# Gate logits of six token groups: row products with sums on VectorE in place of transposes and strip products on TensorE, in a fused retention, gated feed-forward and mixture-of-experts kernel

## The chip, the cores and the metric

One core of one Trainium2 chip. The metric is the device time of one execution in microseconds (us). Three timed executions of the kernel before gave 1068.44, 1069.57 and 1070.39 us; the median is 1069.57.

## The reference, cut to what matters

Three parts follow each other, in float32: a retention (linear attention with a decaying state, 4 x 8 heads x 768 steps x 64) that gives 3072 tokens of 512 numbers; a gated feed-forward layer; and eight experts, of which each token uses one.

```python
x = attention(q, k, v)                      # (3072, 512)
y = ((x @ w_a) * (x @ w_b)) @ w_out         # (3072, 512), 1536 wide inside
logits = y @ w_gate                         # (3072, 8)
e_idx = np.argmax(logits, axis=1)
gate_w = softmax(logits)[arange, e_idx]
eom = 1 / (1 + np.exp(-(y @ w_output_gate)))   # (3072, 8)
out[t] = gate_w[t] * eom[t, e_idx[t]] * (relu(y[t] @ w1[e_idx[t]]) @ w2[e_idx[t]])
```

So each token needs 16 numbers of its `y`: 8 gate logits and 8 output gate logits. They are what the change computes in another way.

## The kernel before, in words

The kernel is written instruction by instruction for each engine, with semaphores between them; each engine's order is the order of the code, and no scheduler moves anything. Three stages follow each other: attention (to about 87 us of the span), feed-forward (to about 713 us), experts.

**Feed-forward.** The tokens go in 8 groups of 384 (`GT`), 3 tiles of 128 (`TG`). The inner 1536 columns go in 12 steps f of 128 (`KF`). TensorE does `up(g, s, f)` (L940 to L954, 24 matmuls on line L952: x times w_b, then x times w_a, each split into high and low parts), then `down(g, f - 1)` (L956 to L972, 9 matmuls on L970). `up` of step f is issued before `down` of step f - 1, so that the other engines have the length of one `up` and one `down` to make the gated product. Per step ScalarE copies b from PSUM (L712), VectorE multiplies `g_sb` = a * b (L896), ScalarE rounds it to `g_hi` (L715), VectorE subtracts `g_lo` (L898). `down` of step f waits for `g_lo` of step f, and `up` of step f for `g_sb` of step f - 2. At f = 3 the next group's x is split (`split_x_hi` L695 on ScalarE, `split_x_lo` L700 on VectorE, four instructions on L703). At a group's end ScalarE copies the three tiles of y to `y_sb` (L733), and SP stores them (L691). SP loads the next x (`load_x`, L290) at a group's start.

**Gate logits.** `y_sb` has tokens on partitions, and a matmul with the gate weights contracts over partitions, so y is transposed first. For the group before, one piece is put between `up` and `down` of each step (L977 to L985): at f = 0, 1, 2 `pe_yT` (L746, four transposes of a tile into bank 7), each copied to `yT_sb` by `dve_yT` (L771); at f = 3 `pe_partial` (L756: four matmuls, one for each 128 rows of the gate weights, each into a strip of 32 partitions), copied by `dve_partial`; at f = 4 `pe_logits` (L765, which adds the four strips and turns the result), copied by `dve_logits` to `L3`, 128 tokens x 3 tiles x 16. This happens for groups 0 to 6, each during the group after it. The last group has its own place in the expert stage.

**Routing.** Short chains of small VectorE instructions on `L3`, each waiting for the one before it (`link`, L801): `dve_choose` (f = 6, 7 instructions), `dve_gate` (f = 7, 6), `dve_scale` (f = 8, 6), `dve_rank` (f = 9, 5). ScalarE gives two exponentials, TensorE two matmuls at f = 8 (`pe_rank`).

Group 0 is apart (it also splits the weights), groups 1 to 6 run in one loop on SP, ScalarE and VectorE (two groups per turn), and group 7 is apart (it also prepares the experts). TensorE's code is unrolled.

## Time and profile before

| | |
|---|---|
| median of 3 timed runs | 1069.57 us (1068.44 to 1070.39) |
| the profiled execution, device time | 1067.78 us |
| its span, first to last instruction | 1066.0 us |
| granted TensorE clock, mean | 0.998 of full speed |
| TensorE (PE) busy | 1042.6 us, 98% |
| VectorE (DVE) busy | 407.7 us, 38% |
| ScalarE (ACT) busy | 293.4 us, 28% |
| share of TensorE in the chain that ended last | 94% |
| DMA, mean over the span | 93 GB/s |

A busy time is the union of an engine's instructions; matmuls overlap, so the mean duration of one (337 ns on L952) is longer than the time from one start to the next. The chain that ended last is followed back from the last instruction, at each step to what released it. "x24" is a run of 24 instructions merged into one row.

### The profile page before, as it was taken

What the parts mean: (1) busy time and instruction counts of PE and PEld (TensorE: products, weight loads), DVE (VectorE), ACT (ScalarE), POOL (GpSimd) and SP (SyncE); (2) the same over time, 40 slices, a digit from 0 to 9 for tenths busy, and PEclk for the clock granted to TensorE, in tenths of its full rate; (3) what the DMA queues carried; (4) which work ended last, traced back from release to release, by engine and by line L of the source; (5) the groups of instructions that cost most, each with busy time, mean ns of one, the idle gap of its engine ahead of it and who ended that gap; (6) DMA issues with size and microseconds to landing.
All of it is one profiled execution on the core that took longest, in us unless ns stands there. A gap on an engine that the chain in (4) does not pass through costs nothing.

```text
span 1066.0 us, 18259 instructions
## 1 busy us (share of the span) xinstructions
PE 1042.6 (98%) x6489; PEld 932.6 (87%) x6490; DVE 407.7 (38%) x800; ACT 293.4 (28%) x550; POOL 110.8 (10%) x108
## 2 busy tenths in 40 slices
PE   6999999999999999999999999999899999999997
PEld 5888999999999999999999999998688888888886
DVE  3445432222223223223223212458445445354542
ACT  2444332212112112122122121331334334243431
POOL 4770000000000000000000000000121111111111
PEclk9999999999999999999999999999999999999999
DMA  9997801001001001001001002200744433335311
GB/s 364 363 336 224 200 1 61 1 1 60 1 1 60 1 1 60 1 1 60 1 20 41 1 30 79 79 21 32 276 144 146 176 116 118 115 132 198 115 35 35
DMA packets 34091, 98.69 MB, mean 93 GB/s; under 512 B 4397, under 2 KB 10797, under 8 KB 34032
## 3 DMA queue, kind: packets, MB, share of 16 engines
q1 hardware_dynamic: 28976, 83.17, 23.1%
q0 software_dynamic: 4480, 13.90, 3.8%
q8 instruction: 43, 0.70, 0.3%
q10 hardware_dynamic: 576, 0.79, 0.2%
q14 instruction: 16, 0.13, 0.0%
HBM read 80.54 MB, written 18.09 MB: 93 GB/s over the span
## 4 chain that ended last, share of the span: by engine, by line
PE 94%; DMA 4%; DVE 1%; issue 1%; ACT 0%; POOL 0%; ACTq 0%; DVEq 0%; POOLq 0%
PE bank L952 38%; PE bank L970 19%; PE bank L1310 13%; PE bank L1287 13%; PE bank L1295 2%; PE bank L580 2%; DMA rows<-in_steps 2%; PE bank L633 1%; PE bank L531 1%; DMA xg<-x_dram,idx_gather 1%; PE bank L545 1%; PE bank L753 1%; PE bank L566 1%; DMA qdec_t<-in_consts 1%; PE bank L762 1%
## 5 line engine op out<-in xcount | busy, mean ns | idle before, releaser
L952 PE MATMUL bank<-x_hi,wab_hi 128*128 128x384 f32 x768 | 258.6, 337 | 0.0
L952 PE MATMUL bank<-x_hi,wab_lo 128*128 128x384 f32 x768 | 258.2, 336 | 0.0
L952 PE MATMUL bank<-x_lo,wab_hi 128*128 128x384 f32 x768 | 257.6, 335 | 0.0
L896 DVE TENSOR_TENSOR g_sb<-bank,b_sb 128x384 f32<-128x384 f32 x96 | 53.5, 557 | 368.6 <-PE bank L952 368.6
L952 PEld LDWEIGHTS bank<-x_hi,wab_hi 128*128 128x128 f32 x768 | 144.7, 188 | 3.9 <-issue 0.2
L952 PEld LDWEIGHTS bank<-x_lo,wab_hi 128*128 128x128 f32 x768 | 144.5, 188 | 3.7
L952 PEld LDWEIGHTS bank<-x_hi,wab_lo 128*128 128x128 f32 x768 | 144.4, 188 | 0.0
L1287 PE MATMUL bank<-w,xe_hi 128*128 (+1 forms) x432 | 136.2, 397 | 1.2 <-DVE xe_lo L642 1.1
L712 ACT COPY b_sb<-bank 128x384 f32<-128x384 f32 x96 | 46.3, 482 | 255.3 <-PE bank L952 255.3
L970 PE MATMUL bank<-wo_hi,g_hi 128*128 128x512 f32 x288 | 116.0, 403 | 0.0
L970 PE MATMUL bank<-wo_hi,g_lo 128*128 128x512 f32 x288 | 113.7, 395 | 0.0
L970 PE MATMUL bank<-wo_lo,g_hi 128*128 128x512 f32 x288 | 113.5, 394 | 0.0
L715 ACT CAST g_hi<-g_sb 128x384 fp32r<-128x384 f32 x96 | 49.2, 513 | 209.7 <-DVE g_sb L896 209.7
L1233 POOL DMA_INDIRECT xg<-x_dram,idx_gather x28 | 29.0, 1035 | 672.9 <-DVE idx_gather L875 630.0
L1287 PEld LDWEIGHTS bank<-w,xe_hi 128*128 128x128 f32 x432 | 78.8, 188 | 17.3 <-issue 2.1
L1310 PE MATMUL bank<-w_hi,hT_hi 128*128 (+1 forms) x216 | 86.9, 402 | 1.3 <-DVE hT_lo L1030 1.3
L1310 PE MATMUL bank<-w_hi,hT_lo 128*128 (+1 forms) x216 | 84.5, 391 | 0.0
L1287 PE MATMUL bank<-w,xe_lo 128*128 (+1 forms) x216 | 84.5, 391 | 0.0
L1310 PE MATMUL bank<-w_lo,hT_hi 128*128 (+1 forms) x216 | 84.2, 390 | 0.0
L898 DVE TENSOR_TENSOR g_lo<-g_sb,g_hi 128x384 fp32r<-128x384 f32 x96 | 53.6, 558 | 55.6 <-ACT g_hi L715 55.6
L970 PEld LDWEIGHTS bank<-wo_hi,g_hi 128*128 128x128 f32 x288 | 54.2, 188 | 13.8 <-issue 4.4
L970 PEld LDWEIGHTS bank<-wo_hi,g_lo 128*128 128x128 f32 x288 | 54.2, 188 | 11.9
(161 smaller groups left out, 1114.3 us busy)
## 6 DMA issues: line engine op xcount, KB each, us to landing
raw<-in_w SPq DMA_DIRECT2D x64, 512.0 KB, 4.8
rows<-in_steps SPq DMA_DIRECT2D x20, 768.0 KB, 7.8
rows<-in_steps SPq DMA_DIRECT2D x24, 256.0 KB, 7.3
wab_raw<-in_weights SPq DMA_DIRECT2D x24, 256.0 KB, 7.7
x_dram<-y_sb SPq DMA_DIRECT2D x8, 768.0 KB, 4.0
xT_dram<-x_all SPq DMA_DIRECT2D x6, 768.0 KB, 11.9
x_raw<-xT_dram SPq DMA_DIRECT2D x6, 768.0 KB, 5.3
wo_raw<-in_weights SPq DMA_DIRECT2D x4, 768.0 KB, 10.0
```

The source lines that it names most:

```text
L531: ins = nc.tensor.matmul(bank[2 * i + o][:, cols], kT[half_p, cols], qT[half_p, cols], start=True, stop=True)
L580: ins = nc.tensor.matmul(out_at(i, p, o), rows[:, c, 3, h * D:(h + 1) * D], probs[j][:, i, h, :], start=False, stop=(i == ROUND - 1 and p ...
L712: nc.scalar.copy(b_sb[:, f % 2], bank[2 * (f % 2) + 1][:, 0:GT]).then_inc(b_read, 1)
L715: nc.scalar.copy(g_hi[:, f % 2], g_sb[:, f % 2]).then_inc(g_hi_done, 1)
L896: nc.vector.tensor_tensor(g_sb[:, f % 2], bank[2 * (f % 2)][:, 0:GT], b_sb[:, f % 2], ALU.mult).then_inc(g_done, 1)
L898: nc.vector.tensor_tensor(g_lo[:, f % 2], g_sb[:, f % 2], g_hi[:, f % 2].bitcast(F32), ALU.subtract).then_inc(g_lo_done, 1)
L952: ins = nc.tensor.matmul(bank[to][:, 0:GT], wab(w, f, j), x[s][:, k, :], start=(k == 0 and m == 0), stop=(k == KD - 1 and m == 2))
L970: ins = nc.tensor.matmul(bank[4 + t], gp[:, f % 2, toks], wo(w, f), start=(f == 0 and m == 0), stop=(f == KF - 1 and m == 2))
L1233: nc.gpsimd.indirect_dma_start(out=xg_first[s] if i < FIRST else xg[s], out_offset=None, in_=x_dram[0:rows_there], in_offset=bass.Indirect ...
L1287: ins = nc.tensor.matmul(bank[o], x[:, s, k, :], w[:, bass.ds(half + (k * FE + o * 512), 512)], start=(k == 0 and m == 0), stop=(k == KD - ...
L1295: ins = nc.tensor.transpose(bank[2 + o][:, k * P:(k + 1) * P], h_sb[:, (4 * o + k) * P:(4 * o + k + 1) * P], ident)
L1310: ins = nc.tensor.matmul(bank[5 + s], h[:, k, :], w[:, bass.ds(half + k * DM, DM)], start=(k == 0 and m == 0), stop=(k == KE - 1 and m == 2))
```

## The change

For token groups 0 to 5, whose logits are computed during groups 1 to 6 (the loop), TensorE no longer takes part. The two outputs of each token are sums over 512 products of its row of y with a row of gate weights, and VectorE computes these directly: `dve_dots` issues 48 instructions per group (16 gate columns e x 3 tiles t), each multiplying the tile `y_sb[:, t]` (128 x 512) by `gate_row`, writing the products away and their sum to one column of `L3`. `DOTS_AT` says how many of the 48 follow each step f: none, 6, 6, 3, 6, 3, 5, 6, 6, 6, 1, none. Each waits for the one two places before it (`dots_done`); the first of each gate column waits for its row.

The gate weights must lie on all partitions for this. In group 0 TensorE transposes the gate weights once (into bank 7), VectorE copies them to `gates_T`, and SP stores them as 16 rows of 512 numbers in the part of `xT_dram` that groups 0 and 1 don't use. In each loop group SP then copies each of the 16 rows to all 128 partitions (256 KB each), through four slots `gate_row`; a row from the fifth on waits until the three products that used its slot are done. The first four stand ahead of `load_x` in SP's queue, the rest behind it.

The steps of routing move: `dve_choose` from f = 6 to 5 (it needs the first 24 products only), `seen` counts from f = 7 to 6, `dve_rank` stays at 9, the output gate (`dve_own_gate`) is at f = 10 and `dve_scale` at 11; ScalarE's two exponentials move to f = 6 and 11. `g_lo` now lies in the place of `g_sb`, so `g_sb` waits for `down` of step f - 2. ScalarE's copy of y at a group's end waits for all 48 products. Group 6 (during group 7) and group 7 keep the way of before.

```diff
--- before.py
+++ after.py
@@ -38,6 +38,9 @@
 PAIRS_MAX = (SLOT_TILES - 1) // 2
 READY = 2
 PARTS = 4
+GATE_SLOTS = 4
+DOTS = 2 * NE * TG
+DOTS_AT = (0, 6, 6, 3, 6, 3, 5, 6, 6, 6, 1, 0)
 PW = KD * FE // PARTS
 W1_SPAN, W2_SPAN = 2 * KD * FE, KE * DM
 
@@ -180,15 +183,23 @@
     small_end = at[0]
     at[0] = small_at
     b_sb = place("b_sb", (P, 2, GT))
+    g_sb_at = at[0]
     g_sb = place("g_sb", (P, 2, GT))
     g_hi = place("g_hi", (P, 2, GT), F32R)
-    g_lo = place("g_lo", (P, 2, GT), F32R)
+    g_lo = place("g_lo", (P, 2, GT), F32R, where=g_sb_at)
+    product_at = at[0]
+    at[0] += 2 * GT * 4
     y_sb = place("y_sb", (P, TG, DM))
     yT_sb_at = at[0]
     yT_sb = place("yT_sb", (P, KD, GT))
     x_raw_at = max(at[0], yT_sb_at + 3 * DM * 4)
     part_sb = place("part_sb", (P, GT), where=x_raw_at + KD * GT * 4)
     x_raw = place("x_raw", (P, TG, KD, P), where=x_raw_at)
+    after_x = x_raw_at + KD * GT * 4
+    gate_row = [place(f"gate_row{n}", (P, DM), where=(yT_sb_at, yT_sb_at + DM * 4, yT_sb_at + 2 * DM * 4, after_x)[n])
+                for n in range(GATE_SLOTS)]
+    products = [place(f"products{n}", (P, DM), where=(product_at, after_x + DM * 4)[n]) for n in range(2)]
+    gates_T = place("gates_T", (P, P), where=after_x + DM * 4)
 
     at[0] = x_raw_at
     id_first = place("id_first", (P, TILES - TG))
...
@@ -605,6 +619,7 @@
 
     AT_PART, AT_LOGITS = TG, TG + 1
     AT_CHOOSE, AT_GATE, AT_SCALE, AT_RANK = 6, 7, 8, 9
+    DOT_CHOOSE, DOT_SEEN, DOT_RANK, DOT_GATE, DOT_SCALE = 5, 6, 9, 10, 11
     LINKS = 19
     AT_FIRST = 10
     AT_W1_HI = {5: (0, 1), 6: (2, 3)}
@@ -672,13 +687,32 @@
             sp.dma_start(raw[:, q * PW:(q + 1) * PW],
                          src[bass.ds(e, 1), :, q * PW:(q + 1) * PW].rearrange("a p c -> (a p) c")).then_inc(into[q], 16)
 
+    gate_rows = x_groups[0].rearrange("p c -> (p c)")[0:2 * NE * DM].rearrange("(e k p) -> k e p", e=2 * NE, k=KD)
+    gate_rows_flat = x_groups[0].rearrange("p c -> (p c)")[0:2 * NE * DM].rearrange("(e c) -> e c", e=2 * NE)
+
+    def store_gates_T(sp):
+        sp.wait_ge(gates_T_read, 1)
+        for k in range(KD):
+            at_k = k * (P // KD)
+            sp.dma_start(gate_rows[k], gates_T[at_k:at_k + 2 * NE]).then_inc(gates_T_out, 16)
+        sp.wait_ge(gates_T_out, 16 * KD)
+
+    def load_gate_rows(sp, g, which):
+        for e in which:
+            if e >= GATE_SLOTS:
+                sp.wait_ge(dots_done, DOTS * (g - 1) + TG * (e - GATE_SLOTS + 1))
+            sp.dma_start(gate_row[e % GATE_SLOTS], gate_rows_flat[e:e + 1].to_broadcast([P, DM])).then_inc(row_in[e % GATE_SLOTS], 16)
+
     def sp_ff(sp):
         def group(g, s, first, last):
             if first:
                 sp_weights(sp)
+                store_gates_T(sp)
             elif not last:
                 sp.wait_ge(x_lo_done, KD * (g + 1))
+                load_gate_rows(sp, g, range(GATE_SLOTS))
                 load_x(sp, g + 1)
+                load_gate_rows(sp, g, range(GATE_SLOTS, 2 * NE))
             else:
 
                 for half in range(2):
@@ -720,15 +754,17 @@
                 if last and f in AT_W1_HI:
                     split_w1(act, True, 0, AT_W1_HI[f])
                 if not first:
-                    if f == AT_GATE:
+                    if f == (AT_GATE if last else DOT_SEEN):
                         act_exp(act, g - 1)
-                    if f == AT_SCALE:
+                    if f == (AT_SCALE if last else DOT_SCALE):
                         act_exp_og(act, g - 1)
             if last:
                 split_w2(act, True, 0, (0, 1, 2))
             act.wait_ge(down_done, KF * (g + 1) + 2)
             if not first:
                 act.wait_ge(x_out, 16 * g)
+                if not last:
+                    act.wait_ge(dots_done, DOTS * g)
             for t in range(TG):
                 nc.scalar.copy(y_sb[:, t, :], bank[4 + t]).then_inc(y_read, 1)
 
@@ -742,20 +778,23 @@
         act.wait_ge(og_done, g + 1)
         nc.scalar.activation(g_oge, g_og, ACT.Exp, scale=-1.0).then_inc(oge_done, 1)
 
+
+    def on_pe(g):
+        return g - (GROUPS - 2)
 
     def pe_yT(pe, g, t):
         pe.wait_ge(y_read, TG * g + t + 1)
         if t == 0:
             pe.wait_ge(rank_read, g + 1)
         else:
-            pe.wait_ge(yT_read, TG * g + t)
+            pe.wait_ge(yT_read, TG * on_pe(g) + t)
         for k in range(KD):
             ins = nc.tensor.transpose(bank[7][:, k * P:(k + 1) * P], y_sb[:, t, k * P:(k + 1) * P], ident)
         ins.then_inc(yT_done, 1)
 
     def pe_partial(pe, g, yT=yT_sb):
 
-        pe.wait_ge(yT_read, TG * (g + 1))
+        pe.wait_ge(yT_read, TG * (on_pe(g) + 1))
         pe.sem_inc(waited, 1)
         for k in range(KD):
             strip = slice(k * (P // KD), (k + 1) * (P // KD))
...
@@ -809,7 +849,10 @@
 
         v = nc.vector
         tiles = bass.ds(g * TG, TG)
-        dve.wait_ge(logit_read, TG * (g + 1) + 1)
+        if isinstance(g, int) and on_pe(g) >= 0:
+            dve.wait_ge(logit_read, TG * (on_pe(g) + 1))
+        else:
+            dve.wait_ge(dots_done, DOTS * g + DOTS // 2)
         link(v.tensor_reduce(g_max, L3[:, :, 0:NE], AX.X, ALU.max))
         v.tensor_tensor(g_sub, L3[:, :, 0:NE], over(g_max, NE), ALU.subtract).then_inc(sub_done, 1)
         link(v.tensor_tensor(g_eq, L3[:, :, 0:NE], over(g_max, NE), ALU.is_equal))
@@ -819,10 +862,18 @@
         link(v.tensor_copy(onehot[:, tiles, :], g_key8))
 
     def dve_gate(dve, g, link):
-
+        dve_own_gate(dve, g, link)
+        dve_seen(dve, g, link)
+
+    def dve_own_gate(dve, g, link):
         v = nc.vector
+        if not (isinstance(g, int) and on_pe(g) >= 0):
+            dve.wait_ge(dots_done, DOTS * (g + 1))
         link(v.tensor_tensor(g_og8, g_key8, L3[:, :, NE:2 * NE], ALU.mult))
         v.tensor_reduce(g_og, g_og8, AX.X, ALU.add).then_inc(og_done, 1)
+
+    def dve_seen(dve, g, link):
+        v = nc.vector
         link(v.tensor_copy(seen[:, 0, :], seen[:, TG, :]))
         for t in range(TG - 1):
             link(v.tensor_tensor(seen[:, t + 1, :], seen[:, t, :], g_key8[:, t, :], ALU.add))
@@ -883,6 +934,20 @@
         ins.then_inc(first_slots_done, 1)
 
     ROUTE_STEPS = {AT_CHOOSE: dve_choose, AT_GATE: dve_gate, AT_SCALE: dve_scale, AT_RANK: dve_rank}
+    DOT_STEPS = {DOT_CHOOSE: dve_choose, DOT_SEEN: dve_seen, DOT_RANK: dve_rank, DOT_GATE: dve_own_gate, DOT_SCALE: dve_scale}
+
+    def dve_dots(dve, g, f):
+
+        for n in range(sum(DOTS_AT[:f]), sum(DOTS_AT[:f + 1])):
+            e, t = n // TG, n % TG
+            if e == 0:
+                dve.wait_ge(y_read, TG * g + t + 1)
+            if t == 0:
+                dve.wait_ge(row_in[e % GATE_SLOTS], 16 * (2 * NE // GATE_SLOTS * g + e // GATE_SLOTS + 1))
+            if n > 1:
+                dve.wait_ge(dots_done, DOTS * g + n - 1)
+            nc.vector.scalar_tensor_tensor(products[n % 2], y_sb[:, t], 1.0, gate_row[e % GATE_SLOTS], ALU.mult, ALU.mult,
+                                           accum_out=L3[:, t, e:e + 1]).then_inc(dots_done, 1)
 
     def dve_ff(dve):
         first_link = linker(dve, 0, first_linked)[0]
@@ -893,6 +958,7 @@
                 n = g * KF + f
                 dve.wait_ge(a_done, n + 1)
                 dve.wait_ge(b_read, n + 1)
+                dve.wait_ge(down_done, n - 1 + 2)
                 nc.vector.tensor_tensor(g_sb[:, f % 2], bank[2 * (f % 2)][:, 0:GT], b_sb[:, f % 2], ALU.mult).then_inc(g_done, 1)
                 dve.wait_ge(g_hi_done, n + 1)
                 nc.vector.tensor_tensor(g_lo[:, f % 2], g_sb[:, f % 2], g_hi[:, f % 2].bitcast(F32),
@@ -901,7 +967,16 @@
                     split_x_lo(dve, g + 1, 1 - s)
                 if first and f + 2 < KF:
                     split_w_lo(dve, f + 2)
-                if not first:
+                if first and f == 0:
+                    dve.wait_ge(gates_T_done, 1)
+                    nc.vector.tensor_copy(gates_T, bank[7][:, 0:P]).then_inc(gates_T_read, 1)
+                if not first and not last:
+                    dve_dots(dve, g - 1, f)
+                    if f in DOT_STEPS:
+                        DOT_STEPS[f](dve, g - 1, link[0])
+                        if f == DOT_SCALE:
+                            assert link[1][0] == LINKS, link[1]
+                if last:
                     if f < TG:
                         dve_yT(dve, g - 1, f)
                     elif f == AT_PART:
...
@@ -974,15 +1048,17 @@
         def group(g, s, first, last):
             for f in range(KF):
                 up(g, s, f)
-                if not first:
+                if first and f == 0:
+                    nc.tensor.transpose(bank[7][:, 0:P], gates_pad.rearrange("p k e -> p (k e)"), ident).then_inc(gates_T_done, 1)
+                if last:
                     if f < TG:
                         pe_yT(pe, g - 1, f)
                     elif f == AT_PART:
                         pe_partial(pe, g - 1)
                     elif f == AT_LOGITS:
                         pe_logits(pe, g - 1)
-                    elif f == AT_SCALE:
-                        pe_rank(pe, g - 1)
+                if not first and f == AT_SCALE:
+                    pe_rank(pe, g - 1)
                 if last and f == AT_FIRST:
                     pe_first_slots(pe)
                 if last and f == KF - 1:
...
```

Left out of the diff are the new semaphores and a constant that is taken off the counts of those semaphores that now count fewer groups (`on_pe`).

TensorE, the end of `up` at f = 0 and the start of `up` at f = 1 in group 1 (L952 is `up`, L753 `pe_yT`). Before:

```order
L952 MATMUL bank<-x_lo,wab_hi 128x384
L952 MATMUL bank<-x_hi,wab_lo 128x384
L753 MATMUL bank<-ident,y_sb 128x128 [waits rank_read,y_read]
L753 MATMUL bank<-ident,y_sb 128x128 x3
L952 MATMUL bank<-x_hi,wab_hi 128x384 [waits g_done]
L952 MATMUL bank<-x_lo,wab_hi 128x384
```

After the change, at the same place (`up` is on L1026):

```order
L1026 MATMUL bank<-x_lo,wab_hi 128x384
L1026 MATMUL bank<-x_hi,wab_lo 128x384
L1026 MATMUL bank<-x_hi,wab_hi 128x384 [waits g_done]
L1026 MATMUL bank<-x_lo,wab_hi 128x384
```

The four transposes are gone, and so are those at f = 1 and 2, the strips at f = 3 and the three matmuls at f = 4.

VectorE, step f = 9 of a loop group, where `dve_rank` follows. Before:

```order
L896 TENSOR_TENSOR g_sb<-bank,b_sb 128x384 [waits b_read,a_done]
L898 TENSOR_TENSOR g_lo<-g_sb,g_hi 128x384 [waits g_hi_done]
L848 TENSOR_TENSOR g_5_65<-bank,g_3_63 128x24 [waits rank_done]
L851 TENSOR_REDUCE g_5_71<-g_5_65 128x3 [waits rank_read]
```

After the change (L962 and L964 make `g_sb` and `g_lo`, L949 is one product with sum, L899 begins `dve_rank`):

```order
L962 TENSOR_TENSOR g_sb<-bank,b_sb 128x384 [waits down_done,b_read,a_done]
L964 TENSOR_TENSOR g_lo<-g_sb,g_hi 128x384 [waits g_hi_done]
L948 REGISTER_ALU
L949 SCALAR_TENSOR_TENSOR products_116,L_59<-y_sb,gate_row_112 128x512 [waits dots_done]
L948 REGISTER_ALU [waits row_in2]
L949 SCALAR_TENSOR_TENSOR products_115,L_59<-y_sb,gate_row_113 128x512 [waits dots_done]
...
L948 REGISTER_ALU [waits row_in3]
L949 SCALAR_TENSOR_TENSOR products_116,L_59<-y_sb,gate_row_114 128x512 [waits dots_done]
L948 REGISTER_ALU
L949 SCALAR_TENSOR_TENSOR products_115,L_59<-y_sb,gate_row_114 128x512 [waits dots_done]
L899 TENSOR_TENSOR g_5_65<-bank,g_3_63 128x24 [waits rank_done]
L902 TENSOR_REDUCE g_5_71<-g_5_65 128x3 [waits rank_read]
```

Six products stand ahead of `dve_rank`, and `g_sb` of the next step comes behind both.

SP, the start of group 1. Before:

```order
L291 ISA [waits x_lo_done]
L291 DMA x_raw<-xT_dram 128x1536
L690 REGISTER_ALU
L691 ISA [waits y_read]
L691 DMA x_dram<-y_sb 128x3x512
```

After the change:

```order
L704 DMA gate_row_111<-xT_dram 128x512 [waits x_lo_done]
L704 DMA gate_row_112<-xT_dram 128x512
L704 DMA gate_row_113<-xT_dram 128x512
L704 DMA gate_row_114<-xT_dram 128x512
L302 ISA
L302 DMA x_raw<-xT_dram 128x1536
L703 ISA
L704 DMA gate_row_111<-xT_dram 128x512 [waits dots_done]
L703 REGISTER_ALU
L704 DMA gate_row_112<-xT_dram 128x512 [waits dots_done]
```

Four rows stand ahead of `x_raw`, and twelve more, each waiting for products, ahead of the store of y.

## Rows read from the trace of the kernel before

**Rows 1.** Page: each engine's busy time, share of span and instructions.

```profile
PE 1042.6 (98%) x6489; PEld 932.6 (87%) x6490; DVE 407.7 (38%) x800; ACT 293.4 (28%) x550; POOL 110.8 (10%) x108
```

**Rows 2.** Page: the chain that ended last, shares by line.

```profile
PE bank L952 38%; PE bank L970 19%; PE bank L1310 13%; PE bank L1287 13%; PE bank L1295 2%; PE bank L580 2%; DMA rows<-in_steps 2%; PE bank L633 1%; PE bank L531 1%; DMA xg<-x_dram,idx_gather 1%; PE bank L545 1%; PE bank L753 1%; PE bank L566 1%; DMA qdec_t<-in_consts 1%; PE bank L762 1%
```

**Rows 3.** Busy in a middle group: length, PE, PEld, DVE, ACT, POOL, clock, DMA.

```profile
315.93:394.43 78.50, 78.50 (x427) 72.88 (x427) 21.24 (x57) 15.39 (x33) 0.00 (x0) 1.00 0.06 21
```

**Rows 4.** The chain in order of time (start, us, what).

```profile
315.93 4.14 PE bank L970 x18
320.06 4.19 PE bank L952 x24
...
394.43 4.16 PE bank L970 x18
```

**Rows 5.** Timeline of VectorE over one middle group (start, us, what).

```profile
324.29 0.56 DVE L896 TENSOR_TENSOR g_sb<-bank,b_sb 128x384 f32<-128x384 f32 x1 [6.63 <-PE bank L952]
325.42 0.56 DVE L898 TENSOR_TENSOR g_lo<-g_sb,g_hi 128x384 fp32r<-128x384 f32 x1 [0.58 <-ACT g_hi L715]
325.90 0.68 DVE L773 COPY yT_sb<-bank 128x512 f32<-128x512 f32 x1
328.90 0.56 DVE L896 TENSOR_TENSOR g_sb<-bank,b_sb 128x384 f32<-128x384 f32 x1 [2.32 <-PE bank L952]
...
335.60 0.56 DVE L896 TENSOR_TENSOR g_sb<-bank,b_sb 128x384 f32<-128x384 f32 x1 [4.40 <-PE bank L952]
...
342.30 0.56 DVE L896 TENSOR_TENSOR g_sb<-bank,b_sb 128x384 f32<-128x384 f32 x1 [4.41 <-PE bank L952]
...
343.91 1.96 DVE L703 TENSOR_TENSOR x_lo<-x_raw,x_hi 128x384 fp32r<-128x384 f32 x4
...
349.54 0.56 DVE L896 TENSOR_TENSOR g_sb<-bank,b_sb 128x384 f32<-128x384 f32 x1 [3.20 <-PE bank L952]
...
356.46 0.56 DVE L896 TENSOR_TENSOR g_sb<-bank,b_sb 128x384 f32<-128x384 f32 x1 [5.11 <-PE bank L952]
...
362.72 0.56 DVE L896 TENSOR_TENSOR g_sb<-bank,b_sb 128x384 f32<-128x384 f32 x1 [4.57 <-PE bank L952]
...
364.34 0.17 DVE L813 TENSOR_REDUCE g<-L 128x3 f32<-128x24 f32 x1
...
365.62 0.18 DVE L819 COPY onehot<-g 128x24 f32 x1
...
375.26 0.56 DVE L896 TENSOR_TENSOR g_sb<-bank,b_sb 128x384 f32<-128x384 f32 x1 [3.58 <-PE bank L952]
...
381.94 0.56 DVE L896 TENSOR_TENSOR g_sb<-bank,b_sb 128x384 f32<-128x384 f32 x1 [3.77 <-PE bank L952]
```

**Rows 6.** Busy by line and shape, VectorE.

```profile
L898 DVE TENSOR_TENSOR g_lo<-g_sb,g_hi 128x384 fp32r<-128x384 f32 x96 | 53.6, 558 | 55.6 <-ACT g_hi L715 55.6
...
L329 DVE TENSOR_TENSOR wo_lo<-wo_raw,wo_hi 128x512 fp32r<-128x512 f32 x12 | 8.2, 684 | 3.7 <-ACT wo_hi L315 3.7
```

**Rows 7.** Timeline of VectorE in the attention stage.

```profile
29.64 2.48 DVE L490 TENSOR_TENSOR probs<-bank,mask_t 128x512 f32<-128x512 f32 x4 [3.60 <-PE bank L531]
```

**Rows 8.** Timeline of ScalarE: y to SBUF at a group's end.

```profile
320.10 1.56 ACT L733 COPY y_sb<-bank 128x512 f32<-128x512 f32 x3 [3.03 <-PE bank L970]
```

**Rows 9.** DMA issues: KB each, median us to landing.

```profile
rows<-in_steps SPq DMA_DIRECT2D x24, 256.0 KB, 7.3
...
x_dram<-y_sb SPq DMA_DIRECT2D x8, 768.0 KB, 4.0
...
x_raw<-xT_dram SPq DMA_DIRECT2D x6, 768.0 KB, 5.3
```

More of the change, by code:

```diff
@@ L599, in build @@
     waited = sem("waited")
+    gates_T_done, gates_T_read, gates_T_out, dots_done = (sem("gates_T_done"), sem("gates_T_read"), sem("gates_T_out"),
+                                                          sem("dots_done"))
+    row_in = [sem(f"row_in{n}") for n in range(GATE_SLOTS)]
     x_out = sem("x_out")
@@ L765, in pe_logits @@
     def pe_logits(pe, g, part=part_sb):
-        pe.wait_ge(part_read, g + 1)
+        pe.wait_ge(part_read, on_pe(g) + 1)
         for t in range(TG):
@@ L771, in dve_yT @@
     def dve_yT(dve, g, t):
-        dve.wait_ge(yT_done, TG * g + t + 1)
+        dve.wait_ge(yT_done, TG * on_pe(g) + t + 1)
         nc.vector.tensor_copy(yT_sb[:, :, t * P:(t + 1) * P], bank[7].rearrange("p (k t) -> p k t", k=KD)).then_inc(yT_read, 1)
     def dve_partial(dve, g, part=part_sb):
-        dve.wait_ge(part_done, g + 1)
+        dve.wait_ge(part_done, on_pe(g) + 1)
         nc.vector.tensor_copy(part, bank[7][:, 0:GT]).then_inc(part_read, 1)
     def dve_logits(dve, g):
-        dve.wait_ge(logit_done, TG * (g + 1))
+        dve.wait_ge(logit_done, TG * (on_pe(g) + 1))
         nc.vector.tensor_copy(L3.rearrange("p t e -> p (t e)"), bank[7][:, 0:TG * 2 * NE]).then_inc(logit_read, TG)
@@ L785, in pe_rank @@
         pe.wait_ge(seen_done, g + 1)
-        pe.wait_ge(logit_read, TG * (g + 1) + 1)
+        if on_pe(GROUPS - 2) <= (on_pe(g) if isinstance(g, int) else -1):
+            pe.wait_ge(logit_read, TG * (on_pe(g) + 1))
         to = bank[7][:, 0:TG * NE]
@@ L934, in pe_ff @@
         pe.sem_inc(down_done, 2)
-        pe.sem_inc(logit_read, 1)
         pe.sem_inc(rank_read, 1)
@@ L1015, in pe_counts @@
         pe.wait_ge(seen_done, GROUPS)
-        pe.wait_ge(logit_read, TG * GROUPS + 1)
+        pe.wait_ge(logit_read, TG * (on_pe(LAST) + 1))
         nc.tensor.matmul(bank[7][:, COUNT:COUNT + NE], ones_t, seen[:, TG, :], start=True, stop=True)
@@ L1040, in dve_route @@
         for t in range(TG):
-            dve.wait_ge(yT_done, TG * LAST + t + 1)
+            dve.wait_ge(yT_done, TG * on_pe(LAST) + t + 1)
             v.tensor_copy(yT_last[:, :, t * P:(t + 1) * P], bank[4 + t].rearrange("p (k t) -> p k t", k=KD)).then_inc(yT_read, 1)
```

## Prediction

> **What bounds the kernel now.** I read the page first: TensorE is busy 98% of the span [rows 1], and the chain that ended last runs through `up` (L952, 38%) and `down` (L970, 19%), with L753 (`pe_yT`) and L762 (`pe_partial`) in it at 1% each [rows 2]. Those two are what the change takes away in six groups. Then one middle group: the 78.50 us from 315.93 to 394.43 are all TensorE busy at clock 1.00, while VectorE is busy for 21.24 and DMA 6% [rows 3]. The chain in order of time repeats with the same period: `down` at 315.93 and again at 394.43 [rows 4]. In such a group time is gained only by taking instructions off TensorE, and VectorE has 57 us to spare, if nothing waits for it.
>
> **What is removed.** The cost of each inserted piece is read from VectorE's `g_sb`, which starts when `up` of its step ends [rows 5]. A step without insert takes 362.72 - 356.46 = 6.26 us: 4.19 for `up` [rows 4], the rest, 2.07, for `down`. From f = 0 to f = 1 there is only one `up` and the first tile's transposes: 328.90 - 324.29 = 4.61, so 0.42 for them. The other two tiles: 335.60 - 328.90 and 342.30 - 335.60, each 6.70, so 0.44 each. The strips: 349.54 - 342.30 = 7.24, so 0.98. The logits: 356.46 - 349.54 = 6.92, so 0.66. Sum 2.94 us. The rank matmuls (381.94 - 375.26 = 6.68, so 0.42) stay. Twelve plain steps, 75.1, with 2.94 and 0.42 make 78.5, the measured period. Six groups give 6 x 2.94 = 17.6 us. The period would be 75.56.
>
> **What is added on TensorE.** One transpose in group 0: a quarter of 0.44, and the stop and restart of the stream. I take 0.2 us. VectorE's copy of it (128 columns) and SP's four stores lie in group 0, where SP has only y to store afterwards; nobody waits for them before the first row is loaded. Zero.
>
> **What is added on VectorE, and when it shows.** The cover is large: `down` of step f needs `g_lo` of step f one plain step, 6.26 us, after the end of `up` f. `g_lo` is ready 1.69 us after `g_sb` starts (325.42 + 0.56 - 324.29), and the next instruction can start at 1.61 (325.90) [rows 5]. So VectorE may be some 4.5 us late before TensorE stands. With a time d from the start of one product to that of the next, a step of six products takes 1.61 + 6d.
>
> No row shows the new instruction. The nearest is the two-source subtraction of 128 x 512 float32, both sources in SBUF like here: 684 ns, against 558 for 384 columns, so 0.98 ns per column [rows 6]. Back to back they overlap: four 512-column products take 2.48 us, so (2.48 - 0.68) / 3 = 0.60 us from start to start [rows 7]. What the sum costs more is unknown. If it comes for nothing, d = 0.60; that is the low end, since every column must still pass. If it is like one more small instruction behind each product, the routing chain prices it: seven from 364.34 to 365.62 + 0.18, 1.46 us, 0.21 each [rows 5]; d = 0.81. If nothing overlaps, 0.684 + 0.17 = 0.85. The high end is a product at half rate: 512 more column times, 0.60 + 0.50 = 1.10, and 1.20 if the whole time doubles. I take 0.75, between the first two, because columns, types and places are those of the 684 ns row.
>
> The longest path through VectorE: f = 1 to 10 without a gap are 10 x 1.61 = 16.1, the 48 products, the four `x_lo` (1.96, from 343.91, less overlap: 1.9), and the routing steps that stay there: `dve_choose` 1.46 and eleven small ones (`seen` 4, rank 5, output gate 2) at 0.21, 3.8. Then f = 11 to the next f = 1 hang on TensorE: `g_sb` and `g_lo` 1.69, `down` 2.07, two `up` 8.38, together 12.1. Sum: 33.9 + 48d. It sets the period only beyond 75.56, that is from d = 0.87; it eats the whole gain (78.5) from d = 0.93. At 0.75 it is 69.9. The densest steps, f = 7, 8 and 9, take 1.61 + 4.5 = 6.1 each at d = 0.75, and 1.0 more at f = 9 for the rank: some 0.9 us late against a cover of 4.5. Hence zero. What is queued behind a product is `g_sb` of the next step; ScalarE's `g_hi` and TensorE's `down` wait for that. The exponentials, moved to f = 6 and 11, find their inputs made a step earlier or, at 11, lie behind `g_hi`. `g_lo` in the place of `g_sb` adds a wait for `down` f - 2, which TensorE issues before the `up` for which `g_sb` waits anyway. The three copies of y that go, 0.68 us each [rows 5], are in steps that the products fill again. If the cover were gone, a dense step would cost what it takes over 6.26 us.
>
> **DMA and SP.** Sixteen rows of 256 KB are 4.2 MB per group, 55 GB/s on queues that are 6% busy now [rows 3]. At the start y is in SBUF at 320.10 + 1.56 = 321.7 [rows 8]; then SP issues the store of y (768 KB, 4.0 us), rows 0 to 3 and x (5.3 us when alone) [rows 9]. The first product wants its row at f = 1, about 330.1, 8.4 us later; if 768 KB need 5.3 us, the store and the first two rows need 8.8 in line, inside 8.4 and the cover. x comes some 7 us later than before, at about 334 to 338; it is wanted at 342. Later rows are asked for nine products ahead; in the dense steps two rows are used per 6.26 us through four slots, so a slot turns in 12.5 us, of which 2.3 are its products. A row may need 10 us. A 256 KB load in the crowded first stage took 7.3 [rows 9]. Zero.
>
> **Sum.** Against the profiled execution, 1067.78: -17.6 + 0.2 gives 1050.4. The median of the timed runs lies 1.8 above the profiled one, 1069.57, so I expect 1052.2.
>
> **The rivals.**
>
> *Products at half rate.* The mechanism: two float32 streams from SBUF and a running sum, one column in two cycles. For it speaks only that no row shows this instruction; against it, that two float32 sources without a sum run at 0.98 ns per column [rows 6]. Then d = 1.10 to 1.20, VectorE is the engine that TensorE waits for in steps 6 to 12, and the period is 33.9 + 48d = 86.7 to 91.5: 6 x 8.2 = 49 to 6 x 13.0 = 78 us more, 1119 to 1148. It decides from d = 0.93 on. The Trainium skill states this very rule: in "Vector Engine (DVE) Microarchitecture Reference", points that are easy to get wrong, this instruction form "with two non-bf16 SBUF sources halves throughput". By that rule the result would be 1119 or more. Nothing in this trace shows whether it holds, and the form without a sum does not show the halving. Chance 0.17, and 0.02 for other ways to over 1072.
>
> *The sum as a second instruction, dearer than taken, or rows late.* With d between 0.87 and 0.93 the gain shrinks by 48 x 0.01 x 6 = 2.9 us for each 0.01. Rows that need 13 us, like a crowded queue, would miss by 3 us at each of two turns of a slot in the dense steps, less the 4.5 of cover: 1.5 us a group, 9 in all, 1061. For it: 96 copies with one source address each, a pattern that the trace lacks. Against it: idle queues. Range 1055 to 1067, chance 0.07. That the sum is a second instruction is what the Trainium skill says ("VectorE: DVE Perf Modes", two Vector instructions with no wait between them: "an op that also writes out its accumulator is two instructions"); by that d would be 0.81 here, and the result still 1052.
>
> *The gain is not one.* The removed pieces could stand where TensorE would have waited for `g_lo`. The rows speak against it: `g_lo` is ready 4.5 us early [rows 5], and TensorE shows no idle time [rows 3]. Then 1067 to 1072, chance 0.04.
>
> **How the numbers follow.** Hidden products: chance 0.70, 1052.2 with 1050 to 1055. Partly hidden: 0.07. No gain: 0.04. Slower: 0.19. A measurement of this kernel tells 0.2%, some 2 us, from no change. The range leaves out the half rate and reaches over the others: 1049.5 to 1068. Faster 0.77, same 0.04, slower 0.19.
>
> **What would show each step right or wrong.** Right: the chain repeats every 75.5 to 75.6 us; from f = 0 to 1 `g_sb` takes 4.2 and all other steps but f = 9 6.26; L753's count falls from 84 to 12. L949 has 288 instructions of 0.65 to 0.85 us. VectorE's busy time in a group is 21.2 - 2.0 + 48 x 0.75, about 55. `down` never waits for `g_lo`. Rows land within 10 us. Wrong: products over 1 us, or an idle time of TensorE before L1044 released by `g_lo`, late in the group (half rate); the first product of a step waiting for a row, with the same idle time behind it (late rows); the period at 75.6 but a longer time elsewhere, in group 0 or the experts, which I price at nothing.

## The result, and the profile after

The changed kernel took 1053.11 us (median of 4 runs, 1050.76 to 1054.60), the kernel before 1069.98 in the same comparison (4 runs, 1068.44 to 1072.87). The ratio is 0.9837, 95% interval 0.9807 to 0.9868: 1.6% faster. Forecast were 1052.2 in a range of 1049.5 to 1068.0. The profiled execution took 1050.76 us against 1050.4 forecast for it, with a span of 1048.9, 17.1 less than before.

The engines, from the page (before: [rows 1]):

```profile
PE 1026.0 (98%) x6334; PEld 920.8 (88%) x6335; DVE 571.3 (54%) x1347; ACT 293.4 (28%) x550; POOL 110.7 (11%) x108
```

TensorE lost 16.6 us of busy time, VectorE gained 163.6, and the end followed TensorE.

One middle group of the changed kernel, to be read like [rows 3] (length; busy time of PE, PEld, DVE, ACT, POOL; clock; DMA share; GB/s):

```profile
310.34:385.92 75.58, 75.58 (x401) 70.86 (x401) 48.47 (x148) 15.40 (x33) 0.00 (x0) 1.00 0.24 77
```

Its length fell from 78.50 to 75.58 us, still filled by TensorE, with VectorE at 48.47 in place of 21.24 and DMA at 24% in place of 6%. The chain in order of time shows the period as in [rows 4]: `down` (now L1044) of f = 10 and 11 at 310.34, 385.92, 461.48 and 537.06, and behind the first of these two `up` without anything between them:

```profile
310.34 4.16 PE bank L1044 x18
314.49 8.34 PE bank L1026 x48
...
385.92 4.14 PE bank L1044 x18
...
461.48 4.16 PE bank L1044 x18
...
537.06 4.18 PE bank L1044 x18
```

VectorE's rows for the new instruction (busy by line and shape: busy us, mean ns, idle time before):

```profile
L949 DVE SCALAR_TENSOR_TENSOR products<-y_sb,gate_row 128x512 f32<-128x512 f32 x288 | 180.9, 688 | 0.0
...
L949 DVE DVE_READ_ACCUMULATOR products<-y_sb,gate_row 128x1 f32 x288 | 24.2, 84 | 0.0
```

The product with sum is two instructions: the product, 688 ns where the plain subtraction of the same shape has 684 [rows 6], and the reading of the sum, 84 ns. Where they fall is seen in VectorE's timeline of one group, from f = 0 to 1 and from f = 8 to 10, where the products are densest (`g_sb` of f = 0, 1, 8, 9, then two products of f = 9, the first and last of the rank steps, and `g_sb` of f = 10):

```profile
318.71 0.56 DVE L962 TENSOR_TENSOR g_sb<-bank,b_sb 128x384 f32<-128x384 f32 x1 [5.45 <-PE bank L1026]
...
322.88 0.56 DVE L962 TENSOR_TENSOR g_sb<-bank,b_sb 128x384 f32<-128x384 f32 x1 [2.46 <-PE bank L1026]
...
366.74 0.56 DVE L962 TENSOR_TENSOR g_sb<-bank,b_sb 128x384 f32<-128x384 f32 x1 [0.89 <-PE bank L1026]
...
373.42 0.56 DVE L962 TENSOR_TENSOR g_sb<-bank,b_sb 128x384 f32<-128x384 f32 x1 [1.31 <-PE bank L1026]
...
375.03 0.69 DVE L949 SCALAR_TENSOR_TENSOR products<-y_sb,gate_row 128x512 f32<-128x512 f32 x1
375.64 0.08 DVE L949 DVE_READ_ACCUMULATOR products<-y_sb,gate_row 128x1 f32 x1
375.64 0.69 DVE L949 SCALAR_TENSOR_TENSOR products<-y_sb,gate_row 128x512 f32<-128x512 f32 x1
...
378.71 0.18 DVE L899 TENSOR_TENSOR g<-bank,g 128x24 f32<-128x24 f32 x1
...
379.56 0.17 DVE L905 TENSOR_SCALAR t_tle<-g_ranki 128x3 int32 x1
379.95 0.56 DVE L962 TENSOR_TENSOR g_sb<-bank,b_sb 128x384 f32<-128x384 f32 x1 [0.22 <-DVE t_tle L905]
```

`g_sb` of f = 1 starts 4.17 us behind that of f = 0 (4.61 in [rows 5]), with no transposes between. At f = 9 the next product starts together with the reading of the sum before it, 0.61 us behind the last one. Behind six products and the rank steps, which end at 379.56 + 0.17, `g_sb` of f = 10 starts at 379.95; a plain step after 373.42 is 379.69, so it is 0.26 late. That is all the lateness in the group, against a cover of 4.5.

The transfers (KB each, median us to landing):

```profile
gate_row<-xT_dram SPq DMA_DIRECT2D x96, 256.0 KB, 3.2
...
x_raw<-xT_dram SPq DMA_DIRECT2D x6, 768.0 KB, 6.8
```

A row of gate weights lands in 3.2 us (6.1 at most); x, which has four of them ahead, in 6.8 in place of 5.3 [rows 9].

### The profile page after: what moved, and what is told of

Its sections match the earlier page's. It is cut to its first block, busy times and chain, and to the rows that moved or that the text cites. A ratio compares the mean times of both kernels' runs of the same rounds, so it can differ in the third digit from the quotient of the medians.

```text
span 1048.9 us, 18935 instructions
## 1 busy us (share of the span) xinstructions
PE 1026.0 (98%) x6334; PEld 920.8 (88%) x6335; DVE 571.3 (54%) x1347; ACT 293.4 (28%) x550; POOL 110.7 (11%) x108
## 4 chain that ended last, share of the span: by engine, by line
PE 94%; DMA 4%; DVE 1%; issue 1%; POOL 0%; ACT 0%; ACTq 0%; DVEq 0%; POOLq 0%
PE bank L1026 38%; PE bank L1044 19%; PE bank L1386 14%; PE bank L1363 13%; PE bank L1371 2%; PE bank L591 2%; DMA rows<-in_steps 2%; PE bank L542 1%; PE bank L648 1%; DMA xg<-x_dram,idx_gather 1%; PE bank L556 1%; DMA qdec_t<-in_consts 1%; PE bank L577 1%; PE bank L932 0%; POOL out L1314 0%
## 5 line engine op out<-in xcount | busy, mean ns | idle before, releaser
L1026 PE MATMUL bank<-x_hi,wab_hi 128*128 128x384 f32 x768 | 257.8, 336 | 0.0
L1026 PE MATMUL bank<-x_hi,wab_lo 128*128 128x384 f32 x768 | 257.7, 336 | 0.0
L1026 PE MATMUL bank<-x_lo,wab_hi 128*128 128x384 f32 x768 | 257.2, 335 | 0.0
L949 DVE SCALAR_TENSOR_TENSOR products<-y_sb,gate_row 128x512 f32<-128x512 f32 x288 | 180.9, 688 | 0.0
L962 DVE TENSOR_TENSOR g_sb<-bank,b_sb 128x384 f32<-128x384 f32 x96 | 53.5, 558 | 186.3 <-PE bank L1026 185.0
L1026 PEld LDWEIGHTS bank<-x_hi,wab_hi 128*128 128x128 f32 x768 | 144.3, 188 | 4.3 <-issue 0.4
L1026 PEld LDWEIGHTS bank<-x_lo,wab_hi 128*128 128x128 f32 x768 | 144.2, 188 | 3.7
L1026 PEld LDWEIGHTS bank<-x_hi,wab_lo 128*128 128x128 f32 x768 | 144.1, 188 | 0.0
L1044 PE MATMUL bank<-wo_hi,g_lo 128*128 128x512 f32 x288 | 114.3, 397 | 0.0
L1044 PE MATMUL bank<-wo_lo,g_hi 128*128 128x512 f32 x288 | 114.2, 396 | 0.0
L1044 PE MATMUL bank<-wo_hi,g_hi 128*128 128x512 f32 x288 | 113.9, 396 | 0.0
L964 DVE TENSOR_TENSOR g_lo<-g_sb,g_hi 128x384 fp32r<-128x384 f32 x96 | 53.6, 558 | 55.7 <-ACT g_hi L749 55.7
L1044 PEld LDWEIGHTS bank<-wo_hi,g_lo 128*128 128x128 f32 x288 | 54.4, 189 | 11.8
```

Source lines behind the costliest of these rows:

```text
L949: nc.vector.scalar_tensor_tensor(products[n % 2], y_sb[:, t], 1.0, gate_row[e % GATE_SLOTS], ALU.mult, ALU.mult, accum_out=L3[:, t, e:e + ...
L962: nc.vector.tensor_tensor(g_sb[:, f % 2], bank[2 * (f % 2)][:, 0:GT], b_sb[:, f % 2], ALU.mult).then_inc(g_done, 1)
L964: nc.vector.tensor_tensor(g_lo[:, f % 2], g_sb[:, f % 2], g_hi[:, f % 2].bitcast(F32), ALU.subtract).then_inc(g_lo_done, 1)
L1026: ins = nc.tensor.matmul(bank[to][:, 0:GT], wab(w, f, j), x[s][:, k, :], start=(k == 0 and m == 0), stop=(k == KD - 1 and m == 2))
L1044: ins = nc.tensor.matmul(bank[4 + t], gp[:, f % 2, toks], wo(w, f), start=(f == 0 and m == 0), stop=(f == KF - 1 and m == 2))
```

## The experiments

Ten runs follow, each beside the kernel before; e9 is the changed kernel once more, and e10 that of e2. The two theories at the start: (T) the gain is TensorE's own time in the removed pieces, and the products are free because VectorE may be 4.5 us late and is not; (R) some of the gain, or a hidden price, is elsewhere: in the copies and waits that went, in VectorE's total, or in the rows. A period is the mean over the six loop groups, taken from ScalarE's first copies of y at the groups' ends.

### e1: TensorE's pieces put back

```diff
+    def pe_idle_pieces(pe, g, f):
+        if f < TG:
+            pe.wait_ge(y_read, TG * g + f + 1)
...
+            for k in range(KD):
+                nc.tensor.transpose(bank[7][:, k * P:(k + 1) * P], y_sb[:, f, k * P:(k + 1) * P], ident)
+        elif f == AT_PART:
+            for k in range(KD):
+                nc.tensor.matmul(bank[7][k * (P // KD):(k + 1) * (P // KD), 0:GT], gates_pad[:, k, :], y_sb[:, k % TG, 0:GT], start=True, stop=True)
+        elif f == AT_LOGITS:
+            for t in range(TG):
+                nc.tensor.matmul(bank[7][:, t * 2 * NE:(t + 1) * 2 * NE], y_sb[:, t, 0:P], sel, start=True, stop=True)
```

> The changed kernel with TensorE's pieces put back where they stood, as work that nobody reads: in the six loop groups 12 transposes of y at f = 0 to 2, four strip products of 384 columns at f = 3 and three of 16 columns at f = 4; VectorE still makes all logits as row products. Theory (the whole gain is TensorE's own time, the products cost nothing): the group period goes back from 75.57 to 78.5 us, 6 x 2.94 = 17.6 us more than the changed kernel, so the time of the kernel before, ratio 0.999 to 1.001. Rival (part of the gain is the waits and copies that went with the pieces, or the products cost something hidden): period clearly off 78.5; 77 or less if the copies carried part of the gain, 79 or more if the products cost something as soon as TensorE has its old work.

Measured: 1068.98 us (12 runs), before 1067.44, ratio 1.0007 (0.9992 to 1.0022). The period is 78.53, against 78.52 in the kernel before; two `down` of the chain:

```profile
316.47 4.14 PE bank L1059 x18
...
394.97 4.16 PE bank L1059 x18
```

So the gain is the time of those matmuls, as far as this comparison can tell. The copies of VectorE that went with them carried no part of it (they are not put back here), and 288 products, 96 row loads and one more transpose together cost less than it can tell: 0.02 us in the period, and at most 0.22% of the whole time by the interval.

### e4 and e5: how late may VectorE be?

```diff
-DOTS_AT = (0, 6, 6, 3, 6, 3, 5, 6, 6, 6, 1, 0)
+DOTS_AT = (0, 6, 6, 3, 6, 3, 5, 14, 4, 0, 1, 0)
```

> The changed kernel with 14 products at f = 7, 4 at f = 8, none at f = 9 in place of 6, 6, 6. The step f = 7 then takes VectorE 1.61 + 14 x 0.613 = 10.2 us against 6.26, so g_sb of f = 8 starts some 4 us late. Theory (cover of 4.5 us until down waits): no change of the time, period 75.57. Rival (a VectorE that is over its step costs TensorE what it is over): 3.9 us per group, 23 us in all.

Measured: 1051.52 us, ratio 0.9835 (0.9809 to 0.9861), period 75.60, the same as the changed kernel's. `g_sb` of f = 7 and of f = 8:

```profile
363.66 0.56 DVE L962 TENSOR_TENSOR g_sb<-bank,b_sb 128x384 f32<-128x384 f32 x1 [0.82 <-PE bank L1026]
...
373.84 0.55 DVE L962 TENSOR_TENSOR g_sb<-bank,b_sb 128x384 f32<-128x384 f32 x1
```

They are 10.18 us apart where a plain step has 6.26: 3.9 us late in every group, and nothing lost. The rival would have cost 23.

In e5 the line reads `5, 18, 0, 0, 1, 0` from f = 6 on.

> The changed kernel with 18 products at f = 7 and none at f = 8 and 9 in place of 6, 6, 6. Step f = 7 takes VectorE 1.61 + 18 x 0.613 = 12.6 us, so g_sb of f = 8 starts 6.4 us late and g_lo with it. Theory (cover of 4.5 us): TensorE waits once per group for g_lo of f = 8, some 1.6 to 1.9 us, 9 to 11 us in all, 1062 to 1064. Rival (no cover): 6.4 us per group, 38 us in all. Rival (more cover than the rows show): no change.

Measured: 1063.02 us, ratio 0.9954 (0.9938 to 0.9971), period 77.32. VectorE, `g_sb` of f = 7 and 8 and `g_lo` of f = 8, then the first `down` of f = 8 on TensorE:

```profile
363.54 0.56 DVE L962 TENSOR_TENSOR g_sb<-bank,b_sb 128x384 f32<-128x384 f32 x1 [0.82 <-PE bank L1026]
...
376.18 0.55 DVE L962 TENSOR_TENSOR g_sb<-bank,b_sb 128x384 f32<-128x384 f32 x1
...
377.31 0.56 DVE L964 TENSOR_TENSOR g_lo<-g_sb,g_hi 128x384 fp32r<-128x384 f32 x1 [0.58 <-ACT g_hi L749]
```

```profile
377.92 0.50 PE L1044 MATMUL bank<-wo_hi,g_hi 128*128 128x512 f32 x1 [1.47 <-DVE g_lo L964]
```

12.64 us apart, 6.4 late, and TensorE stands 1.47 us until `g_lo`; with the stream's restart the period grows by 1.73 (77.33 against 75.60). Of 6.4 us late, some 4.6 were covered, which is the cover read from [rows 5].

### e6 and e7: how many products fit?

```diff
-            if n > 1:
-                dve.wait_ge(dots_done, DOTS * g + n - 1)
-            nc.vector.scalar_tensor_tensor(products[n % 2], y_sb[:, t], 1.0, gate_row[e % GATE_SLOTS], ALU.mult, ALU.mult,
-                                           accum_out=L3[:, t, e:e + 1]).then_inc(dots_done, 1)
+            for r in range(TIMES[e % 2]):
+                c = dots_before(e) + t * TIMES[e % 2] + r
+                if c > 1:
+                    dve.wait_ge(dots_done, DOTS * g + c - 1)
+                nc.vector.scalar_tensor_tensor(products[c % 2], y_sb[:, t], 1.0, gate_row[e % GATE_SLOTS], ALU.mult, ALU.mult,
+                                               accum_out=L3[:, t, e:e + 1] if r == 0 else again[:, c % 2:c % 2 + 1]).then_inc(dots_done, 1)
```

`TIMES` is (1, 2) in e6 and (2, 2) in e7.

> The changed kernel with every product of an odd gate column made twice, the second sum to a place that nobody reads: 72 products per group in place of 48. Theory (the path through VectorE from f = 1 to 10 and back over TensorE, 33.9 + 0.613 x 72 = 78.0 us, sets the period as soon as it is over 75.57): period 78 to 79, some 15 to 21 us more than the changed kernel, 1068 to 1074. Rival (only VectorE's sum per group counts): busy 48.5 + 24 x 0.61 = 63.1 us of 75.6, no change.

Measured: 1071.89 us, ratio 1.0045 (1.0028 to 1.0062), period 78.97. A middle group:

```profile
320.05:398.94 78.89, 76.06 (x402) 70.77 (x401) 62.63 (x196) 14.97 (x34) 0.00 (x0) 1.00 0.24 74
```

VectorE is busy for 62.63 of 78.89 us and sets the period all the same: TensorE stands for 2.8 us of the group.

> The changed kernel with every product made twice, 96 per group, which is also what products at half the rate would have cost. Theory (path 33.9 + 0.613 x 96 = 92.7 us): period 92 to 94, 103 to 109 us more than the changed kernel, 1156 to 1162. Rival (only VectorE's sum counts): busy 77.9 us and 7 of waits for g_hi, period at most 85, at most 57 us more.

Measured: 1164.5 us (2 runs), ratio 1.0909 (1.0887 to 1.0931), period 94.3. A middle group:

```profile
257.14:352.29 95.15, 82.28 (x402) 73.75 (x401) 77.33 (x244) 14.53 (x34) 0.00 (x0) 0.95 0.19 62
```

This is the half rate that was the rival on the slow side, made by hand. The path through VectorE gives 78.0 and 92.7, and the periods are 78.97 and 94.3; VectorE's total gives no change and at most 85, and is refuted. The path is somewhat short. Of e7's times, 1164.5 us lies above the 1156 to 1162 that were expected. The group shown has the granted clock at 0.95, and the rows say where: at its end TensorE stands for 3.66 us, and the 18 `down` behind that take 7.26 us in place of 4.16:

```profile
344.91 7.26 PE bank L1053 x18
...
344.90:349.00 4.10, 4.09 (x10) 0.50 0.00 0
```

The second line is a stretch on TensorE alone (its length, busy, granted clock, DMA share, GB/s). The formula has no term for that. What makes up the 1.0 us of e6, whose clock stays at 1.00, was not tried.

### e3 and e8: fewer slots for the rows

```diff
-GATE_SLOTS = 4
+GATE_SLOTS = 2
```

> The changed kernel with two slots for gate rows in place of four. Theory: a slot turns in three products (1.84 us) and a load of 3.2 us with its issue, some 5.4 us in all, below the 6.26 us in which a dense step uses each slot once, so VectorE waits for no row at a step's start and little within it, and the time stays that of the changed kernel within 1 us. Rival (four slots are what hides the rows): rows come late in the dense steps by more than the cover of 4.5 us, and the period grows by 1 us or more, 6 us or more in all.

Measured: 1051.93 us, ratio 0.9839 (0.9813 to 0.9864), period 75.60. VectorE does wait for rows, 4.1 us in one group (who waited for whom: us in total, times, longest). One such wait is at f = 7, whose `g_sb` starts at 364.39; that of f = 8 starts at 371.22, 0.57 later than a plain step. With two more such waits and the rank steps `g_sb` of f = 10 starts at 385.85, some 2.3 us late:

```profile
DVE products L949 <- DMA gate_row<-xT_dram: 4.1, 3, 1.5
```

```profile
369.99 0.69 DVE L949 SCALAR_TENSOR_TENSOR products<-y_sb,gate_row 128x512 f32<-128x512 f32 x1 [1.45 <-DMA gate_row<-xT_dram]
...
371.22 0.55 DVE L962 TENSOR_TENSOR g_sb<-bank,b_sb 128x384 f32<-128x384 f32 x1
...
385.85 0.56 DVE L962 TENSOR_TENSOR g_sb<-bank,b_sb 128x384 f32<-128x384 f32 x1 [0.22 <-PE bank L1044]
```

The cover takes it all: the period is that of the changed kernel. With four slots VectorE waits for no row.

> The changed kernel with one slot for gate rows: each row is asked for when the three products of the row before are done, so every load of some 3.6 us stands on VectorE's path. Theory: 16 x 1.84 + 15 x 3.6 = 83.4 us for the rows, with f = 11 to f = 1 behind it (12.1) and the first step's 1.6, a period of about 97, some 130 us more than the changed kernel, 1180 or so. Rival (the loads overlap with the rest of VectorE's and TensorE's steps): period below 85.

Measured: 1224.41 us (2 runs), ratio 1.147 (1.1411 to 1.1529), period 104.1 where 97 were expected. Two rows in the chain, and one row's products on VectorE (its first, the `g_sb` between its second and third, and the first of the next row):

```profile
278.84 2.98 DMA gate_row<-xT_dram
...
283.89 3.11 DMA gate_row<-xT_dram
```

```profile
335.92 0.69 DVE L949 SCALAR_TENSOR_TENSOR products<-y_sb,gate_row 128x512 f32<-128x512 f32 x1 [3.24 <-DMA gate_row<-xT_dram]
...
337.14 0.55 DVE L962 TENSOR_TENSOR g_sb<-bank,b_sb 128x384 f32<-128x384 f32 x1
...
342.58 0.69 DVE L949 SCALAR_TENSOR_TENSOR products<-y_sb,gate_row 128x512 f32<-128x512 f32 x1 [3.14 <-DMA gate_row<-xT_dram]
```

The load itself is as short as before, 3 us. A pause for a row is 3.1 to 3.3 in these rows, not 3.6: in this group (103.1 us) the twelve plain turns from row to row take 5.04 to 5.33 us where the sum had 5.44, which makes it 3.5 us shorter. What the sum left out is more than that, and is of two kinds.

The first is seen in the second fence: where a row's products lie on both sides of a step's end, the 1.61 us of `g_sb` and `g_lo` stand ahead of the third one, and the next load is asked for later. Four step ends in a group are such (f = 6 to 9), 6.4 us; the routing steps at two of them, `seen` and rank, add some 2.

The second is on TensorE. Before the last 18 `down` of the group it stands for 5.33 us, and then runs at granted clock 0.50, so that they take 6.07 us in place of 4.16:

```profile
363.99 6.07 PE bank L1044 x18
...
363.90:367.00 3.10, 3.02 (x7) 0.50 0.00 0
```

Hence the way from `g_sb` of f = 11 over TensorE to that of the next f = 1 takes 13.4 us in place of 12.1. Together this makes up the 6 us between 97.1 and this group's 103.1 within some tenths. It is a reading of the trace; no run tests a part of it by itself.

### e2, e9 and e10: the seventh group as well

If VectorE may be late, group 7 has room for products as well: e2 makes those of group 6 there. TensorE's and VectorE's old pieces there are gone, ScalarE's second exponential is at f = 10, and `dve_scale` follows the first slots.

```diff
+DOTS_LAST = (0, 7, 7, 7, 7, 7, 3, 4, 4, 2, 0, 0)
...
+                load_gate_rows(sp, g, range(GATE_SLOTS))
                 for half in range(2):
                     sp.wait_ge(a_done, g * KF + 2 * half + 2)
                     load_expert(sp, raw1, w1_in, 0, raw1_in, (2 * half, 2 * half + 1))
+                    load_gate_rows(sp, g, range(4 + 4 * half, 8 + 4 * half))
...
-        return g - (GROUPS - 2)
+        return g - (GROUPS - 1)
...
+                    dve_dots(dve, g - 1, f, DOTS_LAST)
+                    for step in {6: (dve_choose,), 7: (dve_seen,), 9: (dve_rank, dve_own_gate)}.get(f, ()):
+                        step(dve, g - 1, link[0])
```

> The changed kernel with group 6 treated like groups 0 to 5: its 48 products are made during group 7, at 7 per step for f = 1 to 5 and 3, 4, 4, 2 for f = 6 to 9; no y transposes, strips or logit matmuls in group 7; the output gate at f = 9, the scale at f = 10. Theory (cover of 4.5 us against a product every 0.61 us): another 2.94 us less, about 1050.2 by the median of 1053.1, ratio to before 0.981. Rival (group 7's VectorE, which also splits the first expert's weights and finds its first slots, has no room): TensorE waits for g_lo or for the first slots at f = 10, and the gain is nil or a loss of some us.

Measured: 1045.33 us (before 1067.44), ratio 0.9803 (0.9778 to 0.9828). Group 7 fell from 82.99 to 78.46 us, that is by 4.53 and not 2.94. It has VectorE at 58.26 us:

```profile
615.65:694.11 78.46, 78.46 (x429) 73.77 (x428) 58.26 (x163) 20.37 (x37) 2.21 (x2) 1.00 0.39 125
```

The other 1.6 us are the clock behind the 21 narrow matmuls for the first slots (L881 before, 2 columns each), which end at 704.7 us in the kernel before, at 687.4 in the changed kernel and at 683.2 in e2. TensorE in the kernel before (stretch, its length, busy, granted clock, DMA share, GB/s):

```profile
702.00:704.50 2.50, 2.50 (x25) 1.00 0.00 0
704.50:707.50 3.00, 3.00 (x12) 0.75 0.00 0
707.50:710.00 2.50, 2.50 (x11) 0.62 0.42 116
```

In the changed kernel:

```profile
685.00:687.40 2.40, 2.40 (x23) 1.00 0.00 0
687.40:691.20 3.80, 3.80 (x12) 0.55 0.01 4
691.20:695.40 4.20, 4.20 (x26) 1.00 0.46 125
```

In e2, at the same place:

```profile
680.70:683.20 2.50, 2.50 (x24) 1.00 0.00 0
683.20:685.40 2.20, 2.20 (x11) 1.00 0.00 0
```

In the first two the clock falls to its lower level, 1.2 GHz, for some 3 us (0.55 over 3.8 us), and the nine matmuls of `down` at 687.40 take 3.75 us in place of 2.08; in e2 they take 2.17. To see whether that is chance, the changed kernel and that of e2 were run again side by side.

> The changed kernel unaltered, timed beside e10 on one chip, with a new profile. Theory: ratio to before 0.984, group period 75.57. Open is group 7: in the first profile down of f = 9, which follows the 21 narrow matmuls for the first slots, took 3.7 us in place of 2.08 at granted clock 0.55; before and e1 have the same dip there, e2 has not. If the dip belongs to the place it is there again.

Measured: 1050.0 us (before 1068.99), ratio 0.9825 (0.9803 to 0.9847). Group 7 is 82.99 us again, and the nine `down` take 3.75.

> The kernel of e2 again, beside e9. Theory (only TensorE's removed time counts): 2.94 us less than e9, ratio to before 0.981. If the dip of the clock behind the narrow matmuls stays away here as it did in e2, 4.5 us less, ratio 0.980, and group 7 is 78.5 us long; if it comes back, group 7 is 80.1.

Measured: 1047.99 us, ratio 0.9806 (0.9782 to 0.9830). Group 7 is 78.45, the nine `down` take 2.17. In nine of the ten profiles that keep group 7's old pieces (before, the changed kernel, e1, e3 to e7, e9) the group is 82.98 to 83.04 us long; in the two without them it is 78.5. That looks as if the dip went with the order of work of group 7, but the tenth profile speaks against it. In e8 group 7 has the same instructions as in the changed kernel (only the groups before it run otherwise), and the same 21 narrow matmuls end at 857.3 us. The granted clock stays at 1.00, the nine `down` take 2.17 us, and the group is 81.41 us long (TensorE alone; in the changed kernel first, then in e8):

```profile
616.94:699.93 82.99, 82.99 (x455) 0.98 0.21 67
...
786.85:868.26 81.41, 81.41 (x455) 1.00 0.21 69
...
857.32 2.17 PE bank L1044 x9
```

So the old pieces don't always bring the dip, and two profiles without it don't show that their absence prevents it. When it comes, it does not begin at a fixed place either: in the kernel before the first five `down` behind the narrow matmuls are still at full speed (start to start 0.23 to 0.32 us), in the changed kernel already the first is slow (0.44). What decides stays open. What the removed pieces themselves are worth is seen with the dip left out: 81.41 (e8) less 78.45 (e10) is 2.96 us, the 2.94 forecast. The kernel of e2 is the fastest of the study; between it and e9 the medians differ by 2.0 us and the ratios' intervals overlap, so that it beats the changed kernel rests on group 7 in the profiles: some 2.9 us there are removed work, and 1.6 are there only as long as the dip stays away.

## Why the prediction was right

**The bound and what was removed.** Right. Forecast were 2.94 us per group and a period of 75.56; measured are 75.6 and 2.92 per group (ends of group 0 and 6: 471.09 us apart before, 453.60 after). e1 shows that this is TensorE's own time. From f = 0 to 1 it is 4.17 us (4.2 forecast), and the step with the rank matmuls is unchanged (373.42 - 366.74 = 6.68).

**The added transpose.** Right: group 0's part from the first `up` to its end went from 75.38 (163.07 - 87.69) to 75.58 us, the 0.2 taken. It was a guess of the right size; no run tests it by itself.

**The price of a product.** Mis-sized on the safe side: 0.75 us from start to start was taken, 0.61 measured, next to the low end of 0.60. The reading of the sum is an instruction of its own, as the Trainium skill says ("VectorE: DVE Perf Modes", two Vector instructions with no wait between them), but it begins with the next product and costs 0.01 us, not the 0.21 of the chained small ones: those wait for each other, and each product waits for the one two places before it. That this is the reason was not tried. Hence VectorE was busy for 48.5 us in a group, not 55, and 0.3 us late at most, not 0.9.

**The half rate.** It did not come. Two float32 sources in SBUF and a sum: 688 ns for 512 columns, where half rate would have been near 1.2 us. The Trainium skill's rule ("Vector Engine (DVE) Microarchitecture Reference", points that are easy to get wrong), by which the result would have been 1119 or more, does not hold for this instruction here; the measurement decides. The chance of 0.17 that I gave it was for a form that the trace did not contain. What the rival would have cost was right in kind and somewhat low in size: e7 gives 1164.5 for what amounts to a product at 1.23 us, where the text had 1119 to 1148 for 1.10 to 1.20 (33.9 + 48 x 1.23 would be 92.9, measured 94.3; the clock behind TensorE's stands is not in the formula).

**Cover and path.** The cover is right, and now shown: 4.5 us by the rows, some 4.6 by e5. The path is right in kind: break-even was put at 33.9 + 48d = 78.5, and e6, with 72 x 0.613 = 44.1 in place of the 44.6 at break-even, came out 0.45% slower than before: the formula is short by about 1 us per group.

**DMA.** Right in that nothing waited. The rows landed in 3.2 us, not the 7.3 of the crowded stage; x took 1.5 us longer from its issue to landing and was issued 2.7 us later in the group (319.98 - 314.61 against 322.81 - 320.10), 4.2 us in all and not 7, and the slowest row took 6.1 us where 10 were allowed. e3 shows that half the slots do.

**The sum.** 1050.4 forecast and 1050.76 measured for the profiled execution; by the median 0.9 us off, within the spread of the runs. So good a hit of the whole time is in part luck, since the medians themselves move by 2 us and more between comparisons (the kernel before 1067.44 to 1069.98, the changed kernel 1050.0 to 1053.11); what bears the mechanism out is the period, and e1, e4 and e5.
